# Loading kv in rows of 8 KB per partition and pooling it with parts of a band matrix

## The reference

```python
kv_pool = kv.reshape(B, H // 4, 4, W // 4, 4, C).mean(axis=(2, 4))   # 96 x 8 = 768 keys
kv_flat = kv_pool.reshape(B, -1, C) @ w_sr                           # k = v = kv_flat
a = softmax(q @ k.T / sqrt(C));  x = a @ v
h = x @ w_in1;  x = (where h > 0: h, else alpha * h) @ w_out1        # 2048 hidden columns
h = x @ w_in2;  g = (a0 + a1 h + a2 h^2 + a3 h^3) / (1 + |b0||h| + |b1| h^2 + 1e-6)
out = g @ w_out2
```

## Time and profile before

| What | us |
|---|---|
| median of 3 runs (1547.93 to 1549.79) | 1547.98 |
| the profiled execution's own time | 1547.8 |
| its span in the trace | 1546.0 |
| PE busy | 1508.4 |
| DVE busy | 1433.9 |
| ACT busy | 1401.4 |
| start of the first score product | 34.08 |

### The profile page before, as it was taken

How to read it: one execution, slowest core, us unless ns; L and a number is a source line. 1 busy time by engine, 2 the same in 40 slices (tenths; PEclk the granted TensorE clock), 3 DMA queues, 4 the chain that set the end, 5 groups by cost and what they waited for, 6 DMA issues and landing times. The chain is left out here.

```text
span 1546.0 us, 28282 instructions
## 1 busy us (share of the span) xinstructions
PE 1508.4 (98%) x8269; PEld 1247.6 (81%) x8269; DVE 1433.9 (93%) x2260; ACT 1401.4 (91%) x2714; POOL 1230.5 (80%) x1346
## 2 busy tenths in 40 slices
PE   6999999999999999999999999999999999999986
PEld 5899999867888888888888888888888888888875
DVE  4788888739999999999999999999999999999998
ACT  1677777749999999999999999999999999999997
POOL 0444444408999999999999999999999999999997
PEclk9999999999999999999999999999999999999998
DMA  8100010000000000000000000000000000000000
GB/s 247 54 24 22 29 48 21 1 1 1 8 8 1 8 8 8 8 1 8 8 8 1 8 8 8 8 1 8 8 8 1 8 8 8 8 1 8 8 8 8
DMA packets 12330, 24.94 MB, mean 16 GB/s; under 512 B 1536, under 2 KB 1680, under 8 KB 11920
## 3 DMA queue, kind: packets, MB, share of 16 engines
q1 hardware_dynamic: 11424, 22.55, 4.7%
q10 hardware_dynamic: 752, 0.60, 0.1%
HBM read 16.85 MB, written 6.29 MB: 15 GB/s over the span
## 5 line engine op out<-in xcount | busy, mean ns | idle before, releaser
L285 POOL TENSOR_TENSOR cubic<-sq,lin_p 128x512 f32<-128x512 f32 x384 | 495.1, 1289 | 75.1 <-ACT sq L560 48.5
L276 POOL TENSOR_TENSOR rational<-newton,ratio 128x512 f32<-128x512 f32 x333 | 429.7, 1291 | 30.8 <-PE banks L1544 21.3
L1544 PEld LDWEIGHTS banks<-wout,rational 128*128 128x128 f32 x3072 | 403.0, 194 | 41.1 <-issue 10.6
L1544 PE MATMUL banks<-wout,rational 128*128 128x128 f32 x3072 | 405.4, 277 | 1.9 <-POOL rational L276 1.4
L1345 PE MATMUL banks<-x_hi,win_lo 128*128 128x512 f32 x768 | 387.8, 505 | 15.0 <-DVE ratio L1054 12.6
L1347 PE MATMUL banks<-x_hi,win_hi 128*128 128x512 f32 x768 | 303.3, 395 | 0.0
L1346 PE MATMUL banks<-x_lo,win_hi 128*128 128x512 f32 x768 | 302.6, 394 | 0.0
L578 ACT ACTIVATE lin_p<-banks,ab_raw 128x512 f32<-128x512 f32 x384 | 294.4, 767 | 3.8 <-PE banks L1347 3.8
L1037 DVE SCALAR_TENSOR_TENSOR banks<-sq,abs_b,banks 128x512 f32<-128x512 f32 x384 | 286.5, 746 | 3.5 <-ACT banks L570 3.1
L1045 DVE SCALAR_TENSOR_TENSOR banks<-banks,ab_raw,cubic 128x512 f32<-128x512 f32 x384 | 287.9, 750 | 0.0
L1054 DVE SCALAR_TENSOR_TENSOR ratio<-banks,ab_raw,rcp 128x512 f32<-128x512 f32 x384 | 285.2, 743 | 1.6 <-POOL rational L276 0.2
(11 more groups left out here) (91 smaller groups left out, 2305.7 us busy)
## 6 DMA issues: line engine op xcount, KB each, us to landing
early<-in_kv_dram SPq DMA_DIRECT2D x24, 256.0 KB, 9.4
out_dram<-y_out SPq DMA_DIRECT2D x24, 256.0 KB, 2.0
neg_part<-in_q_dram SPq DMA_DIRECT2D x22, 256.0 KB, 2.7
early<-in_moe_w_in_dram SPq DMA_DIRECT2D x1, 1024.0 KB, 14.2
wout<-in_moe_w_in_dram SPq DMA_DIRECT2D x1, 1024.0 KB, 5.3
neg_part<-in_q_dram ACTq DMA_DIRECT2D x2, 256.0 KB, 8.9
early<-in_w_sr_dram ACTq DMA_DIRECT2D x1, 64.0 KB, 2.0
wout<-in_moe_w_out_dram SPq DMA_DIRECT2D x2, 0.5 KB, 12.2
```

Source lines behind the costliest of these rows:

```text
L276: nc.gpsimd.tensor_tensor(rational[:, m % 3, :], newton[:, m % 2, :], ratio[:, m % 2, :], ALU.mult).then_inc(s["rat_done"], 1)
L285: nc.gpsimd.tensor_tensor(cubic[:, m % 2, :], sq[:, m % 2, :], lin_p[:, m % 2, :], ALU.mult).then_inc(s["cubic_done"], 1)
L1544: last = nc.tensor.matmul(banks[:, ACC2, t * P:(t + 1) * P], rational[:, m % 3, t * P:(t + 1) * P], wout2[:, c, :], start=(c == 0 and t == ...
```

## The change

kv is loaded in rows of 8 KB. A chunk's tile now has an image row on each partition: 128 image rows by 16 of the 32 pixels of a row. Chunks 1 to 4 are one DMA of 1 MB each, chunks 0 and 5 two DMAs of 512 KB, so there are eight instead of 24. A chunk again holds 128 keys: 32 groups of four image rows by four groups of four pixels. The latter are its four units.

Summing over four image rows is now a sum over partitions. It is done on PE by a product with a band matrix: `row_sums(u)` is a window of 128 columns into `spread`, which is zero but for 32 columns that hold one for each group of four partitions; the window's place puts the result at unit u's 32 keys. For some units (`BY_DVE_UNITS`) DVE first sums the four pixels in a 128x512 reduction, and PE needs one product; for the others PE does four, one for each pixel. DVE makes `spread`'s 32 columns from the identity before the first chunk, after a memset on POOL.

The queries of groups 0 and 1 go from ACT's queue to SP's, behind chunks 1 and 2. The two coefficient loads go from ACT's queue to SP's, behind w_out1. ACT's `abs_b` goes from the start to the phase change near 320 us. Alpha's transpose goes behind chunk 0 on PE, `one_minus_al` behind chunk 1 on DVE.

```diff
+    kv_rows = kv[0].rearrange("(k h) (n w) c -> k n h (w c)", h=P, n=2)
+    CELLS = P // POOL_SIDE            # 32
+    UNITS = P // CELLS                # 4
+        BY_DVE_UNITS = ((0, 2), (0, 1), (0, 1, 2), (0, 1, 2), (0, 1), (0, 2))
 # SP
-            for c in range(CHUNKS):
-                for r in range(POOL_SIDE):
-                    sp.dma_start(kv_in[:, c, r * POOL_SIDE * P:(r + 1) * POOL_SIDE * P],
-                                 kv_rows[c * key_rows:(c + 1) * key_rows, :, r, :])...
+            half = UNITS // 2 * POOL_SIDE * P
+            sp.dma_start(kv_in[:, 0, 0:half], kv_rows[0, 0, :, 0:half]).then_inc(s["ld_kv0"], 16)
+            sp.dma_start(kv_in[:, 0, half:], kv_rows[0, 0, :, half:]).then_inc(s["ld_kv_first"], 16)
+            for c in range(1, CHUNKS - 1):
+                sp.dma_start(kv_in[:, c, :], kv_rows[c // 2, c % 2]).then_inc(s[f"ld_kv{c}"], 16)
+                if c <= 2:
+                    sp.dma_start(q_in[:, c - 1, :], q_groups[c - 1]).then_inc(s[f"ld_q{c - 1}"], 16)
+            sp.dma_start(kv_in[:, CHUNKS - 1, 0:half], ...).then_inc(s[f"ld_kv{CHUNKS - 1}"], 16)
+            sp.dma_start(kv_in[:, CHUNKS - 1, half:], ...).then_inc(s["ld_kv_rest"], 16)
             sp.dma_start(raw_in[0], w_in1).then_inc(s["ld_in1"], 16)
             sp.dma_start(wout1[:], ...).then_inc(s["ld_out1"], 16)
+            sp.dma_start(ab_raw[:, 0:4], coef_p.partition_broadcast(P)).then_inc(s["ld_ab"], 16)
+            sp.dma_start(ab_raw[:, 4:6], coef_q.partition_broadcast(P)).then_inc(s["ld_ab"], 16)
 # POOL
+            nc.gpsimd.memset(spread, 0.0).then_inc(s["spread0"], 1)
 # ACT: coefficient and query DMAs removed; abs_b moved to the phase change
-            copy_pooled_t(0); query_hi(0); copy_pooled_t(1); query_hi(1); copy_pooled_t(2)
+            copy_pooled_t(0); copy_pooled_t(1); query_hi(0); copy_pooled_t(2); query_hi(1)
...
-            act.wait_ge(s["cols_done"], 1)
+            act.wait_ge(s["ld_ab"], 32)
+            nc.scalar.activation(abs_b[:], ab_raw[:, 4:6], ACT.Abs).then_inc(s["absb_col_done"], 1)
+            act.wait_ge(s["absb_col_done"], 1)
 # DVE
-                nc.vector.tensor_reduce(pooled[:, c, :], kv_in[:, c, 0:DVE_PIXELS * P]..., AX.X, ALU.add)
+                for u in BY_DVE_UNITS[c]:
+                    pixels = kv_in[:, c, u * POOL_SIDE * P:(u + 1) * POOL_SIDE * P]
+                    nc.vector.tensor_reduce(pooled[:, c, u, :], pixels.rearrange("p (x n) -> p n x", x=POOL_SIDE),
+                                            AX.X, ALU.add).then_inc(s["pooled_done"], 1)
+            nc.vector.tensor_reduce(spread[:, P - CELLS:P], ident[:].rearrange("p (n r) -> p n r", r=POOL_SIDE),
+                                    AX.X, ALU.add).then_inc(s["row_sums_done"], 1)
+            pool_keys(1); one_minus_al; pool_keys(2); query_lo(0); pool_keys(3); query_lo(1); pool_keys(4)
-            pool_keys(1); query_lo(0); pool_keys(2); query_lo(1); pool_keys(3); pool_keys(4)
 # PE
-                for j in range(DVE_PIXELS, PIXELS):
-                    nc.tensor.matmul(dst, kv_in[:, c, j * P:(j + 1) * P], ident[:], ...)
-                nc.tensor.matmul(dst, pooled[:, c, :], ident[:], start=False, stop=True)
+                for u in by_pe:
+                    for x in range(POOL_SIDE):
+                        at = (u * POOL_SIDE + x) * P
+                        nc.tensor.matmul(banks[:, POOLED[c], 0:P], kv_in[:, c, at:at + P], row_sums(u), ...)
+                for n, u in enumerate(BY_DVE_UNITS[c]):
+                    pe.wait_ge(s["pooled_done"], made_before + n + 1)
+                    last = nc.tensor.matmul(banks[:, POOLED[c], 0:P], pooled[:, c, u, :], row_sums(u), ...)
+            pooled_transpose(0); turn_alpha(); pooled_transpose(1); key_chunk(0); queries(0)
+            pooled_transpose(2); key_chunk(1); queries(1)
```

More of the change, by code:

```diff
@@ L100, in build @@
         w_in1_t = early[:, tokens // 2 + ff:tokens // 2 + 2 * ff].rearrange("p (b c) -> p b c", b=BLOCKS)
-        pooled = early[:, 0:keys].rearrange("p (c n) -> p c n", c=CHUNKS)
-        w_sr_sb = early[:, keys:keys + P]
-        al_rows = early[0:BLOCKS, keys + P:keys + 2 * P]
+        w_sr_sb = early[:, 0:P]
+        al_rows = early[0:BLOCKS, P:2 * P]
+        spread = early[:, 2 * P:4 * P]
+        pooled = early[:, 4 * P:4 * P + CHUNKS * UNITS * P].rearrange("p (c u n) -> p c u n", c=CHUNKS, u=UNITS)
         q_in = neg_part
@@ L120, in build @@
         for name in (
-            *(f"ld_kv{c}{part}" for c in range(CHUNKS) for part in "ab"), "ld_wsr", "ld_in1", "ld_out1", "ld_in2", "ld_out2", "ld_al", "ld_ab", "ld_q0", "ld_q1", "st_out",
+            *(f"ld_kv{c}" for c in range(CHUNKS)), "ld_kv_first", "ld_kv_rest", "spread0", "row_sums_done", "ld_wsr", "ld_in1", "ld_out1", "ld_in2", "ld_out2", "ld_al", "ld_ab", "ld_q0", "ld_q1", "st_out",
             "ident0", "absb_col_done", "al_ready", "ident_ready", "pooled_done", "pooled_t_ready", "pooled_t_copied", "k_ready", "k_hi_done", "k_lo_done",
@@ L499, in _ @@
             copy_pooled_t(0)
+            copy_pooled_t(1)
             query_hi(0)
-            copy_pooled_t(1)
+            copy_pooled_t(2)
             query_hi(1)
-            copy_pooled_t(2)
             copy_pooled_t(3)
@@ L904, in pool_keys @@
             def pool_keys(c):
[L906 to L909, removed]
+                dve.wait_ge(s[f"ld_kv{c}"], 16)
+                for u in BY_DVE_UNITS[c]:
+                    if c == 0 and u >= UNITS // 2:
+                        dve.wait_ge(s["ld_kv_first"], 16)
+                    if c == CHUNKS - 1 and u >= UNITS // 2:
+                        dve.wait_ge(s["ld_kv_rest"], 16)
+                    pixels = kv_in[:, c, u * POOL_SIDE * P:(u + 1) * POOL_SIDE * P]
+                    nc.vector.tensor_reduce(pooled[:, c, u, :], pixels.rearrange("p (x n) -> p n x", x=POOL_SIDE),
+                                            AX.X, ALU.add).then_inc(s["pooled_done"], 1)
             def keys_lo(h):
@@ L991, in _ @@
             pool_keys(1)
+            dve.wait_ge(s["al_ready"], 1)
+            nc.vector.tensor_scalar(one_minus_al[:], banks[:, 7, 0:BLOCKS], -1.0, 1.0, ALU.mult, ALU.add).then_inc(s["cols_done"], 1)
+            pool_keys(2)
             query_lo(0)
-            pool_keys(2)
+            pool_keys(3)
             query_lo(1)
-            pool_keys(3)
             pool_keys(4)
@@ L1030, in _ @@
                     scale_out1(g - SCALE_STEP)
+            dve.wait_ge(s["ld_ab"], 32)
+            dve.wait_ge(s["absb_col_done"], 1)
             def denominator(g, c):
@@ L1349, in _, with turn_alpha, row_sums @@
             pe.wait_ge(s["ident_ready"], 1)
-            pe.wait_ge(s["ld_al"], 16)
-            nc.tensor.transpose(banks[:, 7, 0:BLOCKS], al_rows, ident[0:BLOCKS, 0:BLOCKS]).then_inc(s["al_ready"], 1)
+            def turn_alpha():
+                pe.wait_ge(s["ld_al"], 16)
+                nc.tensor.transpose(banks[:, 7, 0:BLOCKS], al_rows, ident[0:BLOCKS, 0:BLOCKS]).then_inc(s["al_ready"], 1)
+            def row_sums(u):
+                first = P - CELLS - u * CELLS
+                return spread[:, first:first + P]
             def pooled_transpose(c):
-                dst = banks[:, POOLED[c], 0:P]
+                by_pe = [u for u in range(UNITS) if u not in BY_DVE_UNITS[c]]
+                made_before = sum(len(units) for units in BY_DVE_UNITS[:c])
                 if c == 4:
@@ L1360, in pooled_transpose @@
                     pe.wait_ge(s["pooled_t_copied"], 1)
-                pe.wait_ge(s[f"ld_kv{c}b"], 32)
-                for j in range(DVE_PIXELS, PIXELS):
-                    nc.tensor.matmul(dst, kv_in[:, c, j * P:(j + 1) * P], ident[:], start=(j == DVE_PIXELS), stop=False)
-                pe.wait_ge(s["pooled_done"], c + 1)
-                nc.tensor.matmul(dst, pooled[:, c, :], ident[:], start=False, stop=True).then_inc(s["pooled_t_ready"], 1)
+                pe.wait_ge(s[f"ld_kv{c}"], 16)
+                if c == 0:
+                    pe.wait_ge(s["row_sums_done"], 1)
+                for u in by_pe:
+                    if c == 0 and u >= UNITS // 2:
+                        pe.wait_ge(s["ld_kv_first"], 16)
+                    if c == CHUNKS - 1 and u >= UNITS // 2:
+                        pe.wait_ge(s["ld_kv_rest"], 16)
+                    for x in range(POOL_SIDE):
+                        at = (u * POOL_SIDE + x) * P
+                        nc.tensor.matmul(banks[:, POOLED[c], 0:P], kv_in[:, c, at:at + P], row_sums(u),
+                                         start=(u == by_pe[0] and x == 0), stop=False)
+                for n, u in enumerate(BY_DVE_UNITS[c]):
+                    pe.wait_ge(s["pooled_done"], made_before + n + 1)
+                    last = nc.tensor.matmul(banks[:, POOLED[c], 0:P], pooled[:, c, u, :], row_sums(u),
+                                            start=False, stop=(n == len(BY_DVE_UNITS[c]) - 1))
+                last.then_inc(s["pooled_t_ready"], 1)
             def key_chunk(c):
```

(7 more changed lines are left out.)

19 lines of the change are left out of this document (5 added, 14 removed).

## The result

| | before | after |
|---|---|---|
| median of 6 runs each, us | 1549.14 (1547.93 to 1550.4) | 1540.28 (1538.38 to 1541.17) |
| ratio, 95% interval | | 0.9939 (0.9929 to 0.995) |
| profiled execution: time, span | 1547.8, 1546.0 | 1541.17, 1539.4 |
| first score product | 34.08 | 26.37 |
| first relu on ACT | 320.93 | 313.91 |

The change makes the kernel 8.9 us faster. A second set, five runs of the changed kernel beside nine of the kernel before, gave 1540.11 against 1550.15, 0.9937 (0.9924 to 0.9951).

The account below looks back on a forecast made before the run. PE bounds the kernel from attention on; before it, the load phase is a transfer with 4.3 us of work behind. 5.9 us from earlier scores less 0.3 for abs_b gives 5.6, so 1542.4 us; range 1540.8 to 1545.9.

Parts of the forecast that it names:

- The chain of the load phase: Before attention: load until chunk 2, DVE's sums until chunk 3, PE's work, tail of 2.23; scores at 28.2, 5.9 us earlier.
- The landings: Load phase: first 0.5 MB lands at 5.5 us, chunk 2 at 13.0, chunk 3 at 16.4, chunk 5 at 20.4 and 21.8.
- I take their mean, 386: Load rate in GB/s for kv in 8 KB rows, mean of 378 and 394 from w_in's stretches; bounds 296 and 430.
- rival A: kv load: row size does nothing, rate stays 296 GB/s; gain 3.5 us, time 1544.5; chance 0.14.
- The coefficient loads: Front of ACT's queue, 4 to 7 us: moving them away wins 2 us of the load phase.
- DVE's sums: Load phase: fourteen sums of 128x512 priced by elements, 1.02 us each; lower end 0.95, extreme 1.90.
- B: Rival on DVE in the load phase: sums cost 1.37 us each; gain 2.7 us, time 1545.3; chance 0.16.
- C: Rival on DVE: a sum costs by its results, 1.90 us as now; 3.0 us slower, 1551.0; chance 0.03.
- key and values 0.93: PE, end of chunk 3: key and value products take 0.93 us, from 20.2 to 21.1.
- PE's products: Load phase: 54 products before and after, 0.233 us each, 0.436 in the first chunk.
- The slow first stretch: PE, first chunk: products at 0.436 us each; lasting beyond chunk 1 would cost 2 us per further chunk.
- abs_b: ACT, before the first relu at the phase change: 0.20 us plus a semaphore costs 0.3 us, bounds 0 and 0.35.

Follow-up runs that it names:

- rows_2k: The changed kernel, but kv read in pieces of 2 KB, at most 512 KB to a DMA (12 DMAs for kv); 1542.17 us, ratio 0.9948.
- old_pattern: The changed kernel with the 24 kv DMAs of the kernel before (16 by 8 rows of 2 KB), wrong pixels pooled, for time alone; 1547.25 us.
- rows_turned: unit_dmas with each DMA's rows going to partitions in another order, as a 16 by 8 source; wrong rows pooled, for time alone; 1548.14 us.
- coef_front: The changed kernel, but the two coefficient loads issued from ACT's queue behind alpha, as before; 1542.70 us, ratio 0.9957.
- unit_dmas: The changed kernel, but kv in 24 DMAs of 256 KB, one per chunk and unit, rows of 2 KB 16 KB apart; 1542.36 us.
- contiguous: unit_dmas, but each DMA reads one 256 KB block lying together in memory; wrong pixels pooled, for time alone; 1540.25 us.

## Why the prediction was right or wrong

**The bound and the way the time goes: right.** PE stays 99.6% busy from 50 to 305 us, and a shift of the first score product by 7.71 us arrives at x_hi near 312 as 7.73. The chain of the load phase is the one worked out: load until chunk 2, DVE's sums until chunk 3's end, PE's own work from there, tail of 2.21 (2.23 forecast).

**The landings: the step that failed.** Chunk 2 landed at 11.85 instead of 13.0, the largest part of the 1.83 us by which the scores began earlier than forecast. 0.67 us of it is the first landing, which I put at 5.5 with no row for how much one DMA in place of two would bring; it came at 4.83. The other 0.48 is the rate: "I take their mean, 386" was too low, 420 measured. The rate that I took from w_in's rows was right to 8%, but its reason was not. I ascribed the 296 to the 2 KB rows. rows_2k moves 390 with such rows, and old_pattern and rows_turned, with a source of 16 by 8, move 278 and 255. The two stretches that I compared differ in both, and I read only one. Of the Trainium skill's rule (DMA: Bandwidth & Descriptors, Specifications: at least 512 B for full rate), which I held against the rows: 2 KB rows reach 390, 93% of the changed kernel's 420, so it is nearly right here, and the conclusion that I drew from it, rival A's 296, was wrong since the 296 had another cause.

**The range: no room for scatter below.** Its lower end was 430 GB/s and sums of 0.95 us, and scatter was allowed for above only. The forecast of the time was 1542.4, and the median is 2.1 us below it. In the profiled execution it is 1.0: 1.8 from the earlier scores, less 0.4 for abs_b, less 0.4 for the last phase. The other 1.1 is that this execution lay 0.9 above its median, where I had put the median 0.2 above the execution. At 1541.17 the profiled execution itself lies inside the range.

**The start of the gain: one quick profile, and three runs.** The median of the kernel before was 1547.98 from three runs and 1549.14 from six, which adds 1.2 us to the gain and nothing to the error in the time. The 34.08 was taken as the kernel's value, while three profiles have 34.08 to 37.07. Since a quick start and a low time belong to the same execution, this hardly touches the forecast of the time; it is why the gain in the medians is larger than in the profiles.

**The coefficient loads: right,** 2 us forecast, 1.9 to 2.2 in coef_front.

**DVE's sums: right,** 1.02 forecast, 1.029 mean and 0.98 from one to the next in a row. From chunk 2's landing to chunk 3's last sum 6.9 us were forecast and 6.37 passed. Rivals B and C, sums priced by their results, are out. One reading in B was wrong: neg_max's row gives 1024 elements 1.27 us and not 1.07, and B's price would have been about 1.27; the measured 1.03 excludes that too. Of the sums, "key and values 0.93" should be 0.98 by its rows, and C's "3.0 slower" 2.9; neither matters.

**PE's products: right:** 8.3 us from chunk 3's last sum to the scores, 8.15 measured. The slow first stretch did not reach chunk 1 in this profile (16 instructions in 2.05 us from 9.43); in others chunk 1 took up to 3.02 (unit_dmas), and from chunk 2's use to the scores it was still 14.56 us.

**abs_b: mis-sized.** 0.3 forecast, 0.71 measured: the wait for the own result and the register load behind it took 0.5 together and not 0.1. Even the upper bound of 0.35 was too low.

In sum: 5.9 forecast to the first score product and 7.71 in the profile (1.15 from the landings, 0.53 on DVE, 0.15 behind it); 0.3 forecast for abs_b and 0.71 measured; 0.4 given back in the last phase of this execution; and 2.2 more in the medians than in the two profiled executions.

Put together from the experiments, the 9.6 us at the first score product are: 1.9 for the coefficient loads and what is left, 1.0, for the new pooling and order of work, from 35.9 to old_pattern's 32.97; 5.9 from there to the 27.05 of rows_2k and of contiguous, for the source with one dimension (contiguous has as many DMAs as old_pattern, so their number isn't needed for it); and 0.8 for rows of 8 KB in fewer DMAs. The second and third term hold the old load's scatter of 3 us.

## What to carry to other kernels

Try a load with one dimension of 128 rows on the source side first, and take the size of the rows second: here the one was worth 110 GB/s (unit_dmas against old_pattern) and the other, with fewer DMAs, 30. Two stretches of one trace that differ in several things don't price any one of them. And where a phase hangs on a load, profile the kernel before more than once: its rate moved by 10% between three profiled executions and the start of the next phase by 3 us. A range needs room for the scatter of the runs at both ends.

## What the runs showed of the hardware

- Loads of 256 KB in rows of 2 KB moved 391 and 388 GB/s (unit_dmas, contiguous) from a source with one dimension of 128 rows, and 278 and 255 (old_pattern, rows_turned) from one of 16 by 8 rows. unit_dmas and rows_turned read the same bytes with each DMA.
- A full DMA share says nothing of the rate: 255, 278, 391 and 389 GB/s all came with shares between 1.05 and 1.07, and 420 with 1.02.
- While two loads of 2 KB and 1 KB, broadcast to 128 partitions, were under way, all DMA engines together moved 98 to 103 GB/s for 3 us in the three profiles of the kernel before, and 173 in coef_front, where moving them to the front cost 1.9 us.
- A scalar that ACT writes itself and loads into a register costs about 0.7 us on the path, for an instruction of 0.20.
